# Staging weights in memory of later stages, and giving GpSimd every second remainder

## The reference

```
state = zeros(B, H, D, D)                     # delta-rule attention, k_n = k / |k|
for t in range(S):
    y[t] = q[t] @ state
    v_old = k_n[t] @ state
    state = state + beta[t] * outer(k_n[t], v[t] - v_old)

h = x @ w_in                                  # dense block, 384 -> 2048 -> 384
x = (h * sigmoid(h)) @ w_out

skip = x @ w_skip > 0                         # routed block, 8 experts of 384 -> 1024 -> 384
e = argmax(x @ w_gate)
out = x + (prob[e] * (relu(x @ w1[e]) @ w2[e]) where skip else 0)
```

## Time and profile before

| | |
|---|---|
| median of 3 runs | 819.45 us (818.46 to 821.53) |
| profiled execution, its own time | 824.12 us |
| its span | 822.3 us |
| PE busy | 781.2 us, 95% |
| DVE busy | 567.5 us, 69% |
| ACT busy | 360.3 us, 44% |
| POOL busy | 114.0 us, 14% |
| granted PE clock, mean | 0.989 of full |

### The profile page before, as it was taken

One profiled execution on the slowest core, in us unless ns is written; L12 is line 12 of the kernel. 1 busy time (PEld: TensorE's weight loads), 2 busy tenths in 40 slices (PEclk: granted clock), 3 DMA queues, 4 the chain that ended last, 5 costly groups with the idle time before them and its releaser, 6 DMA issues.

```text
span 822.3 us, 28779 instructions
## 1 busy us (share of the span) xinstructions
PE 781.2 (95%) x12083; PEld 713.0 (87%) x12083; DVE 567.5 (69%) x1503; ACT 360.3 (44%) x1024; POOL 114.0 (14%) x287
## 2 busy tenths in 40 slices
PE   5877989999999999999999999999999999999993
PEld 3546878999989998899999999999999989999993
DVE  6969887877588775777867687654423577777751
ACT  3723433434435253453434535343443545656531
POOL 1000000001010010101002010010102153445542
PEclk9988999999999999999999999999999999999998
DMA  8772112121311223113130211211024447665610
GB/s 279 210 248 61 34 57 64 60 93 46 93 47 50 83 66 97 41 49 92 57 102 22 67 47 61 71 42 47 22 69 145 134 153 231 209 208 182 195 35 14
DMA packets 48094, 79.83 MB, mean 97 GB/s; under 512 B 5840, under 2 KB 35498, under 8 KB 47968
## 3 DMA queue, kind: packets, MB, share of 16 engines
q1 hardware_dynamic: 44544, 73.07, 27.7%
q0 software_dynamic: 3424, 4.93, 2.0%
HBM read 67.05 MB, written 13.19 MB: 98 GB/s over the span
## 4 chain that ended last, share of the span: by engine, by line
issue 73%; DMA 12%; POOL 8%; PE 3%; DVE 1%; POOLq 1%; ACT 0%; SPq 0%
DMA id_table<-token,slot 6%; DMA out<-kv_t,ids_all 5%; POOL idle L692 3%; PE psum L1003 2%; POOL id_table L737 2%; POOL out L773 1%; POOL kq_t L747 1%; DMA id_table<-x_sb 1%; POOL kq_t L799 1%; DMA x_sb<-kq 1%; PE psum L859 0%; PE psum L1004 0%; DMA ids_all<-id_table 0%; POOLq L769 0%; SPq L573 0%
## 5 line engine op out<-in xcount | busy, mean ns | idle before, releaser
L1037 PE MATMUL psum<-xt_hi,w_hi 128*128 128x256 f32 x768 | 225.1, 293 | 2.1 <-DVE xt_lo L1578 1.0
L1038 PE MATMUL psum<-xt_lo,w_hi 128*128 128x256 f32 x768 | 216.8, 282 | 0.0
L1039 PE MATMUL psum<-xt_hi,w_lo 128*128 128x256 f32 x768 | 216.6, 282 | 0.0
L1213 ACT ACTIVATE h_raw<-psum 128x256 f32<-128x256 f32 x192 | 73.7, 384 | 319.5 <-PE psum L1039 317.6
L1468 DVE TENSOR_TENSOR h_lo<-h_raw,h_hi 128x256 fp32r<-128x256 f32 x192 | 81.3, 423 | 156.5 <-ACT h_hi L1214 143.8
L1037 PEld LDWEIGHTS psum<-xt_hi,w_hi 128*128 128x128 f32 x768 | 144.5, 188 | 9.6 <-issue 2.2
L1039 PEld LDWEIGHTS psum<-xt_hi,w_lo 128*128 128x128 f32 x768 | 145.6, 190 | 0.0
L1038 PEld LDWEIGHTS psum<-xt_lo,w_hi 128*128 128x128 f32 x768 | 145.1, 189 | 0.0
L1061 PE MATMUL psum<-w_hi,h_hi 128*128 128x394 f32 x384 | 138.3, 360 | 0.8 <-DVE h_lo L1468 0.8
L1063 PE MATMUL psum<-w_hi,h_lo 128*128 128x394 f32 x384 | 131.2, 342 | 0.0
L1062 PE MATMUL psum<-w_lo,h_hi 128*128 128x394 f32 x384 | 131.0, 341 | 0.0
(11 more groups left out here) (187 smaller groups left out, 1094.6 us busy)
## 6 DMA issues: line engine op xcount, KB each, us to landing
kq_t<-kq SPq DMA_DIRECT2D x24, 512.0 KB, 3.5
bp<-moe_w SPq DMA_DIRECT2D x24, 512.0 KB, 5.3
kv_t<-kv SPq DMA_DIRECT2D x24, 384.0 KB, 3.2
bp<-moe_w SPq DMA_DIRECT2D x24, 384.0 KB, 4.6
kd<-kq SPq DMA_DIRECT2D x20, 256.0 KB
x_table<-x_sb SPq DMA_DIRECT2D x13, 392.0 KB, 3.0
out<-x_sb SPq DMA_DIRECT2D x12, 384.0 KB
bp<-moe_w_in SPq DMA_DIRECT2D x6, 512.0 KB, 6.3
```

The costliest lines, as they stand in the source:

```text
L1037: m(out, hi, x_hi, start=first, stop=False)
L1038: m(out, hi, x_lo, start=False, stop=False)
L1039: return m(out, lo, x_hi, start=False, stop=last)
L1213: a_.activation(h_raw[i % 2][:, :], up_ps[i % 2][:, 0:G2], ACT.Silu)
```

## The change

Two areas of memory get a second name for the time before the dense block needs them: `early_x` lies where `xt_hi` and `xt_lo` of both pairs will be, `early_h` where `h_hi` and `h_lo` will be. Two of the four staging buffers move from `bp[1]` into `early_x`; the first third of the transposed `w_out` goes to `early_h`, `early_x` and `h_raw`, the second stays in `bp[2]`, the third goes to `early_x`. `bp[1]` now holds nothing but the masks of step 1, and these wait for no weights and no thirds. `minus` gets memory of its own.

Of the 14 pieces the odd ones (three of 128x1024, four of 128x768) are handled by POOL: a `hold` and one subtraction of two SBUF tensors straight into `w_lo`, counted in `w_pool`. PE and ACT keep the even ones. SP waits for `w_pool` ahead of odd pieces.

The first two thirds of `rows` come behind `turn_back`, the third moves into the first pair's slot 10, the scores from slots 1 to 10 to slots 14 to 23, the first `gram` and `mask` of step 2 six and two slots on. `warm` is gone. SP loads kq and kv of step 2 ahead of the thirds, and kq of step 3 right behind them.

```diff
@@ -108,15 +108,21 @@
-        xt_hi = [sb(f"xt_hi{i}", [P, KD, G2], F32R) for i in range(2)]
-        xt_lo = [sb(f"xt_lo{i}", [P, KD, G2], F32R) for i in range(2)]
+        with nc.sbuf_tensor("early_x", [P, 4 * KD * G2], F32) as early_x:
+            pass
+        xt_parts_of = [[sb(f"xt_{part}{i}", [P, KD, G2], F32R) for part in ("hi", "lo")] for i in range(2)]
+        xt_hi, xt_lo = ([xt_parts_of[i][part] for i in range(2)] for part in range(2))
         h_raw = [sb(f"h_raw{i}", [P, G2]) for i in range(2)]
         RING = 4
+        with nc.sbuf_tensor("early_h", [P, 2 * RING * G2], F32) as early_h:
+            pass
...
-        minus = h_hi[:, 0, 0:P]
+        minus = sb("minus", [P, P], F32R)[:, :]
...
-        stage = bp_half[2:6]
+        stage = [early_x[:, WCH * a:WCH * a + WCH] for a in range(2)] + bp_half[4:6]
...
-        kv_row = kv_t[2][:, :, :].rearrange("p s n -> p (s n)")
-        parts_at = [[(kq_t[2][:, 0:2, :], 0), (kq_t[2][:, 2:4, :], 512), (kv_row[:, 0:512].unsqueeze(1), 1024),
+        parts_at = [[(early_h[:, 0:512].unsqueeze(1), 0), (early_h[:, 512:1024].unsqueeze(1), 512), (early_x[:, 2048:2560].unsqueeze(1), 1024),
                      (h_raw[0][:, :].unsqueeze(1), 1536), (h_raw[1][:, :].unsqueeze(1), 1536 + G2)],
                     [(bp[2][:, 2 * j:2 * j + 2, :], 512 * j) for j in range(TURN)],
-                    [(bp[1][:, 2 * j:2 * j + 2, :], 512 * j) for j in range(TURN)]]
+                    [(early_x[:, 512 * j:512 * j + 512].unsqueeze(1), 512 * j) for j in range(TURN)]]
...
-        SCORES_AT = {1: 0, 4: 1, 7: 2, 10: 3}
+        SCORES_AT = {14: 0, 17: 1, 20: 2, 23: 3}
+        ROWS_AT = {10: 2}
...
-        GRAM_AT = {7: (2, 0), 19: (2, 1), 25: (3, 0)}, {6: (2, 0), 12: (2, 1), 27: (3, 0), 30: (3, 1)}
+        GRAM_AT = {13: (2, 0), 19: (2, 1), 25: (3, 0)}, {6: (2, 0), 12: (2, 1), 27: (3, 0), 30: (3, 1)}
...
-        MASK_AT = {14: (2, 0), 20: (2, 1), 28: (3, 0), 34: (3, 1)}
+        MASK_AT = {16: (2, 0), 20: (2, 1), 28: (3, 0), 34: (3, 1)}
...
-                if k == Q - 3:
-                    for n in range(KD):
-                        s["rows"](n)
             s["turn_back"](0)
+            for k in range(2):
+                s["rows"](k)
             for a in range(2):
                 s["mask"](1, a)
...
-                    if p == 0 and x in (1, 2):
-                        s["warm"](5, WP)
+                    if p == 0 and x in ROWS_AT:
+                        s["rows"](ROWS_AT[x])
...
             def load_weights(i):
-                after(sp, w_rest, i - NSTAGE + 1)
+                after(sp, w_pool if i % 2 else w_rest, (i - NSTAGE) // 2 + 1)
...
             def load_rows(k):
                 if k:
-                    sp.wait_ge(w_rest, (WP - 2, WP)[k - 1])
+                    for used in (w_rest, w_pool):
+                        sp.wait_ge(used, (WP // 2 - 1, WP // 2)[k - 1])
...
+            load_kq(2)
+            load_kv(2)
             sp.wait_ge(tables_ready, 1)
...
             for k in range(KD):
                 load_rows(k)
+            load_kq(3)
             sp.dma_start(id_table.rearrange("(p n) a -> p (n a)", p=P), nowhere).then_inc(table_blank, 16)
-            sp.wait_ge(rows_used, 1)
-            load_kq(2)
-            load_kv(2)
...
+            def weights(i):
+                if i % 2:
+                    _, width, _ = piece_of((w_in, w_out), (0, 1), i, PIECES, F, 0)
+                    hi, lo = chunks(w_hi, i), chunks(w_lo, i)
+                    hold(w_half, i + 1)
+                    g.tensor_tensor(lo, stage[i % NSTAGE][:, 0:width].rearrange("p (m n) -> p m n", n=hi.shape[2]), f32(hi), ALU.subtract).then_inc(w_pool, 1)
...
-            schedule(steps(turn=turn, place=place, first=first))
+            schedule(steps(weights=weights, turn=turn, place=place, first=first))
...
                 if t == 1:
                     if a == 0:
-                        pe.wait_ge(w_split, WP)
+                        pe.wait_ge(w_split, WP // 2)
...
             def weights(i):
+                if i % 2:
+                    return
                 _, width, _ = piece_of((w_in, w_out), (0, 1), i, PIECES, F, 0)
                 pe.wait_ge(w_half, i + 1)
-                after(pe, w_split, i - 1)
+                after(pe, w_split, i // 2 - 1)
...
-            def warm(n, weights_done):
-                pe.wait_ge(w_split, weights_done)
-                for _ in range(n):
-                    m(up_ps[1][:, 0:G2], w_hi[0][:, 0:P], w_hi[0][:, 0:G2], start=True, stop=True)
...
             def weights(i):
                 _, width, _ = piece_of((w_in, w_out), (0, 1), i, PIECES, F, 0)
                 act.wait_ge(w_loaded[i % NSTAGE], 16 * (i // NSTAGE + 1))
                 hi = chunks(w_hi, i)
                 cp(hi, stage[i % NSTAGE][:, 0:width].rearrange("p (m n) -> p m n", n=hi.shape[2])).then_inc(w_half, 1)
-                if i >= 1:
+                if i % 2:
                     rest_of(i - 1)
-                if i == WP - 1:
-                    rest_of(i)
...
                 if a == 0:
                     after(dve, pu_done, t - NB + 1)
-                    if t == 1:
-                        dve.wait_ge(w_rest, WP)
-                        dve.wait_ge(rows_used, KD)
                     if t == 2:
                         dve.wait_ge(rows_used, 2)
```

More of the change, by code:

```diff
@@ L517, in steps @@
             names += ["mask", "diag", "evict", "squares", "norms", "spread", "begin", "scales", "gram", "turn", "lanes", "turn_back", "weights", "up", "lo", "down",
-                      "queries", "outputs", "rows", "scores", "first", "split", "x2", "choose", "rank", "place", "warm"]
+                      "queries", "outputs", "rows", "scores", "first", "split", "x2", "choose", "rank", "place"]
             assert set(given) <= set(names)
@@ L637, in _ @@
                 if t + 3 < T:
-                    load_kq(t + 3)
+                    if p:
+                        load_kq(t + 3)
                     load_kv(t + 3)
@@ L659, in expert_weights @@
                     sp.dma_start(dst, src).then_inc(ew_loaded[n], 16)
-            sp.wait_ge(w_split, WP)
+            sp.wait_ge(w_split, WP // 2)
+            sp.wait_ge(w_pool, WP // 2)
             sp.wait_ge(pu_done, T)
@@ L1001, in weights @@
                 for a in range(2):
-                    bank = psum[:, 2 * (i % 2) + a, 0:half]
+                    bank = psum[:, i % 4 + a, 0:half]
                     m(bank, ident[:, :], stage[i % NSTAGE][:, half * a:half * a + half], start=True, stop=False)
@@ L1018, in rows @@
                     pe.wait_ge(route_in, 32)
-                    pe.wait_ge(w_split, WP)
+                    pe.wait_ge(w_split, WP // 2)
+                    pe.wait_ge(w_pool, WP // 2)
                 pe.wait_ge(rows_in[k], 16 * len(turned[k]))
@@ L1023, in rows @@
                     j = at // n
-                    last = m(psum[Q * j:Q * j + Q, 0, at - n * j:at - n * j + x.shape[1]], w_route[:, k, :], x,
+                    last = m(psum[Q * j:Q * j + Q, 1, at - n * j:at - n * j + x.shape[1]], w_route[:, k, :], x,
                              start=k == 0 and at % n == 0, stop=k == KD - 1, skip_group_check=True)
@@ L1031, in turn_scores @@
                     for i in range(TURN):
-                        last = tr(psum[:, 0, P * i:P * i + P], score_row[:, P * i:P * i + P], ident[:, :])
+                        last = tr(psum[:, 1, P * i:P * i + P], score_row[:, P * i:P * i + P], ident[:, :])
                     last.then_inc(score_done, 1)
@@ L1109, in _ @@
             schedule(steps(first=first, place=place, diag=diag, gram=gram, read=read, solve=solve, carry=carry, update=update, outputs=outputs, weights=weights,
-                           queries=queries, up=up, down=down, rows=rows, scores=turn_scores, rank=rank_of, warm=warm))
+                           queries=queries, up=up, down=down, rows=rows, scores=turn_scores, rank=rank_of))
             def transposes(t, a):
@@ L1192, in rest_of @@
                 _, width, _ = piece_of((w_in, w_out), (0, 1), i, PIECES, F, 0)
-                act.wait_ge(w_rest, i + 1)
+                act.wait_ge(w_rest, i // 2 + 1)
                 lo = chunks(w_lo, i)
-                cp(lo, psum[:, 2 * (i % 2):2 * (i % 2) + 2, 0:width // 2].rearrange("p b (m n) -> p (b m) n", n=lo.shape[2])).then_inc(w_split, 1)
+                cp(lo, psum[:, i % 4:i % 4 + 2, 0:width // 2].rearrange("p b (m n) -> p (b m) n", n=lo.shape[2])).then_inc(w_split, 1)
             def weights(i):
@@ L1234, in split_scores @@
                     act.wait_ge(diag_done, 8)
[L1235 removed]
+                    cp(score_row, psum[:, 1, 0:F // TURN]).then_inc(score_copied, 1)
                 if n == 2:
                     act.wait_ge(score_done, 1)
[L1238 removed]
+                    act.wait_ge(w_split, WP // 2)
+                    act.wait_ge(w_pool, WP // 2)
                     cp(scores(w_hi), score_ps).then_inc(score_hi, 1)
```

6 lines of the change are left out of this document (2 added, 4 removed).

## The result

| | before | after |
|---|---|---|
| median of 4 runs each | 819.89 us (818.46 to 821.53) | 826.58 us (825.52 to 828.4) |
| profiled execution, its own time | 824.12 us | 826.97 us |
| its span | 822.3 us | 823.7 us |
| granted PE clock, mean | 0.989 | 0.973 |

The ratio is 1.0095 [1.0075, 1.0114]: slower. The medians differ by 6.7 us, which is 0.8%.

What follows compares the result with a forecast made beforehand. DVE's full work list was taken to set the first dense matmul, after which PE binds. Terms +4.1 (`carry`), +0.3 (clock), +0.5 (`rows`, scores) gave +4.9 us on the 819.45 us median: 824.4 us, range 815.5 to 830.

Steps and rivals of the forecast that it cites:

- The mechanism: Before the dense start, POOL's subtractions and DVE's two-operand instructions exclude each other for whole instructions, both ways: 10.9 us on DVE.
- Rival 1: DVE's lanes before the dense start are not held up by POOL: -5.9 us, 813.6 us, chance 0.14.
- The size of one subtraction: POOL's odd weight pieces: 1.90 us at 1024 wide, 1.47 us at 768, from twice the one-operand copy's pace.
- the change of hands: At each POOL piece that meets DVE: 0.2 us added for this and the `hold`.
- POOL's constants: Later constants on POOL, about 2 us, needed only by the gate's load near 40 us: no cost.
- X: POOL's cost on DVE before the dense start: `carry` comes at 56.5 + X, whole difference X - 6.0 us.
- The holes closed: DVE's waits before the second evict (1.91 us, for PE) and step 1's masks (4.08 us, for third `rows` group) go.
- `carry`: First `carry`, 0.8 us behind the masks before, would follow them directly at 67.4 us: +4.1 us.
- Clock and `rows` behind `carry`: Between first `carry` and dense start: 0.3 us for a lower PE clock, 0.5 us for moved `rows` and scores.
- Rival 3: PE's clock stays at 0.5 until the dense start: about 5 us more, 829.3 us; chance 0.14 shared with another rival.
- The sum: At the first dense matmul: 4.1 + 0.3 + 0.5 = +4.9 us, so it starts near 81.5 us.
- a shift of the dense start is a shift of the end: From the first dense matmul PE is hardly idle, so its shift moves the 822.3 us span's end equally.

Runs made afterwards that it cites:

- POOL alone: The kernel before with only the odd weight pieces given to POOL, other order and memory unchanged: 826.88 us, ratio 1.0102.
- POOL twice: The kernel after with each POOL subtraction but the first made twice in a row: 835.42 us in one execution, span 833.7 us.
- second profile: The kernel before, run again unchanged: 819.71 us, span 817.7 us, front (first evict to first dense matmul) 61.91 us.
- the copy: The kernel after with POOL's seven subtractions replaced by copies of the staged piece into `w_lo`: 819.49 us in one execution.
- both warm ones: 18 idle matmuls added to the kernel with only the memory moves (818.3 us, 0.9985) and to that with DVE's second evict also later (817.49 us, 0.9973).

## Why the forecast came out as it did

**The mechanism** was the one forecast. POOL's subtractions stop DVE's two-operand instructions for their whole length, six of the seven, and the first is free beside the reduction and the transpose. Rival 1 (DVE not held up) would have shown lanes of 0.2 to 0.4 us and 813.6 us. It is refuted by the rows, by POOL alone (1.0102) and by POOL twice. The page's rule, "SBUF — State Buffer" of the Trainium skill, section "SBUF: two separate sides", agrees with these rows in both directions.

**The size of one subtraction** was too low: I took 1.90 and 1.47 us, and they measured 2.35 and 1.66. The stretch is 2.2 and 1.5 us each, so the six cost 10.5 us, where the sum had 10.9 with its 0.2 us a piece for the change of hands. This error cancelled: behind POOL's end the stretched instruction takes only 0.05 to 0.27 us, less than the 0.16 to 0.41 us that it needs alone, so a stretch is up to 0.2 us shorter than the subtraction. The estimate from "GPSIMD Engine Reference" of the Trainium skill, section "Elementwise — side-by-side cycle accounting", 2.25 and 1.69 us, was nearer than mine to the single instruction.

**POOL's constants** I cost at nothing, with the gate's load in mind and not DVE. They took 1.74 us. This is the term that failed: X was 12.3, not 10.9. With the constants ahead, 1.42 of the 1.74 us are gone.

**The holes closed**, 1.9 + 4.08 us, came from one execution. The second profile has 3.58 + 0.72 = 4.3 us. By it the masks should end 12.3 - 4.3 = 8.0 us later; measured from the evict it is 7.6 (55.90 against 48.29).

**`carry`** stood 0.8 us behind the masks in the earlier trace rows, and I took that off. In the second profile it stands 0.15 us behind them, as in after: nothing to gain.

**Clock and `rows` behind `carry`**: I added 0.8 us; it is 14.8 us from `carry` to the dense start in after (66.51 to 81.29) and 13.5 in before (63.30 to 76.79): +1.3. `carry` takes 0.87 against 0.55 us, the third group 1.94. Rival 3, 5 us through the clock, did not come.

**The sum.** Forecast +4.9 us at the dense start. Against the second profile of before: 1.4 more for POOL (12.3 against 10.9), 1.7 for holes that were not there, 0.7 for `carry`, 0.5 behind it, together 9.2; the front measured +8.9. Then the start of the evict gives back 1.7 (a draw) and the rest 1.2, of which 0.9 is PE's gap that after does not have: +6.0, which is 823.7 - 817.7. The medians differ by 6.7. So the absolute 81.5 against 81.29 was partly luck: the first profile of before had the late front, and after an early evict. And "a shift of the dense start is a shift of the end" holds only within 1 to 3 us, because the first stage depends on clock and gap.

Open are the rest without the stage (693.9 to 694.6 us in ten profiles, 693.0 in that of the copy, 695.5 to 696.0 in the first of before and both warm ones), most of the spread of 5 us between executions of one kernel, and why the clock falls at the dense start in some executions and not in others.

## What to carry to other kernels

- Work handed to GpSimd is not free because GpSimd is idle. Ask what VectorE is doing at that moment: if its list is full of instructions with two SBUF operands and it sets the end, each GpSimd instruction that reads SBUF is added to its list at nearly full length (2.2 of the 2.35 us for 1024 elements here). Put such work beside instructions with a PSUM operand, a reduction or a transpose, where it cost 0 to 0.6 us.
- Taking work off an engine that mostly waits (TensorE, 9 us here) gains next to nothing: with POOL only writing, the front is 60.35 us against 60.85 with all pieces on TensorE. And the emptier engine ran at a lower clock (0.66 against 1.00 in 30 to 52 us).
- One profile of the kernel before is one draw: a hole of 4.08 us was 0.72 in the next. Before counting on a hole that ends with a transfer, look at a second execution.

## What was not expected of the hardware

- A stretched VectorE instruction shows no idle time: 0.16 us of lane reads as 2.44 us of busy time. DVE busy rose from 567.5 to 579.0 us with the list unchanged, and the wait is in that number.
- GpSimd instructions that only write (constants, fills of 0.94 and 0.73 us) leave two-operand lanes alone but stretch short one-operand instructions: 0.13 to 1.87 us, 0.18 to 1.15 us. (Lanes were seen beside fills only, not beside the constants.)
- PE has an "issue" gap of 0.84 to 1.61 us at a fixed count of its instructions; ten or 18 matmuls more ahead of it move it by ten or 18.
- The one-element product `hold` took 0.43 us in place of 0.18 where it met a two-operand instruction of DVE (the scale of `kv_t` at 29.77). So each of the two engines waits for the other.
- The two-operand GpSimd subtraction costs (2.35 - 1.66) / 256 = 2.7 ns an element at the margin, the copy (1.03 - 0.81) / 256 = 0.86 ns: three times as much for the second operand, not twice.
